# A chunked linear recurrence with its chunk loops written out and its transposes in another order

## The reference, cut to what matters

```
r, k, v, w, a, b: (batch 4, heads 8, seq 768, dim 40)
for t in range(768):
    y[t]  = r_t @ state                       # state: 40 x 40 per batch and head
    Sa    = state @ a_t
    state = state * w_t - outer(Sa, b_t) + outer(v_t, k_t)
x   = y as (3072, 320)
P   = exp(x @ w_gate - max), normalised by rows and columns 8 times
x   = sum over 8 experts of P[:, e] * (relu(x @ w1[e]) @ w2[e])    # inner width 1024
out = elu(x @ w_in) @ w_out                                        # inner width 2048
```

## Time and profile before

| | |
|---|---|
| Median of 3 runs | 2286.55 us (2280.87 to 2287.19) |
| The profiled execution | 2284.05 us, of which the span is 2282.2 |
| Recurrence | from 0 to about 504 us |
| Gate and experts, second layer | about 512 to 2282 us |
| TensorE busy | 2223.5 us (97% of the span) |
| VectorE, ScalarE, GpSimd busy | 1121.3, 617.4, 176.5 us |

### The profile page before, as it was taken

One profiled execution on the slowest core, in us unless ns is written; L12 is line 12 of the kernel. 1 busy time (PEld: TensorE's weight loads), 2 busy tenths in 40 slices (PEclk: granted clock), 3 DMA queues, 4 the chain that ended last, 5 costly groups with the idle time before them and its releaser, 6 DMA issues.

```text
span 2282.2 us, 37511 instructions
## 1 busy us (share of the span) xinstructions
PE 2223.5 (97%) x14896; PEld 2003.6 (88%) x14896; DVE 1121.3 (49%) x2067; ACT 617.4 (27%) x1113; POOL 176.5 (8%) x194
## 2 busy tenths in 40 slices
PE   7999999979999999999999999999999999999999
PEld 6898888868899998998998998998998998999998
DVE  6776676764363433333333333333333334766665
ACT  3433333323221121221221221221221222433333
POOL 3433333320000000000000000000000000000000
PEclk9999999999999999999999999999999999999999
DMA  5332332322000000100000000000100000000001
GB/s 98 60 59 48 62 60 52 57 55 82 26 26 1 26 26 1 26 26 1 26 26 1 26 15 12 26 2 25 26 1 26 26 1 26 26 1 26 1 12 58
DMA packets 184149, 67.54 MB, mean 30 GB/s; under 512 B 153008, under 2 KB 174000, under 8 KB 183984
## 3 DMA queue, kind: packets, MB, share of 16 engines
q1 hardware_dynamic: 183984, 65.04, 12.2%
HBM read 57.16 MB, written 7.86 MB: 28 GB/s over the span
## 4 chain that ended last, share of the span: by engine, by line
PE 90%; issue 5%; POOL 3%; DVE 2%; ACT 0%; POOLq 0%; DVEq 0%; ACTq 0%
PE up L1099 39%; PE yps L1114 12%; PE yps L1113 12%; PE yps L1112 12%; PE misc L920 4%; PE yps L878 2%; PE up L893 1%; POOL kt L549 1%; PE up L854 1%; PE up L878 1%; PE up L901 1%; PE misc L913 1%; POOL bt L547 1%; PE yps L834 1%; DVE winv L1189 1%
## 5 line engine op out<-in xcount | busy, mean ns | idle before, releaser
L1457 DVE SCALAR_TENSOR_TENSOR hl<-up,hh 128x512 fp32r<-128x512 f32 x384 | 265.5, 691 | 875.7 <-ACT hh L675 875.6
L1114 PE MATMUL yps<-w2h,hl 128*128 128x320 f32 x1920 | 592.7, 309 | 0.0
L1113 PE MATMUL yps<-w2l,hh 128*128 128x320 f32 x1920 | 591.7, 308 | 0.0
L1112 PE MATMUL yps<-w2h,hh 128*128 128x320 f32 x1920 | 591.2, 308 | 0.0
L675 ACT ACTIVATE hh<-up 128x512 fp32r<-128x512 f32 x384 | 229.5, 598 | 1104.2 <-PE up L1099 1104.2
L1099 PE MATMUL up<-xh,w1h 128*128 128x512 f32 x960 | 381.9, 398 | 11.5 <-issue 6.4
L1099 PE MATMUL up<-xl,w1h 128*128 128x512 f32 x960 | 379.5, 395 | 0.0
L1112 PEld LDWEIGHTS yps<-w2h,hh 128*128 128x128 f32 x1920 | 360.6, 188 | 20.4
L1113 PEld LDWEIGHTS yps<-w2l,hh 128*128 128x128 f32 x1920 | 360.5, 188 | 20.4
L1099 PE MATMUL up<-xh,w1l 128*128 128x512 f32 x960 | 377.0, 393 | 0.0
L1114 PEld LDWEIGHTS yps<-w2h,hl 128*128 128x128 f32 x1920 | 360.3, 188 | 0.0
(11 more groups left out here) (189 smaller groups left out, 2211.4 us busy)
## 6 DMA issues: line engine op xcount, KB each, us to landing
w_raw<-in_moe_w SPq DMA_DIRECT2D x16, 640.0 KB, 5.7
w_raw<-in_moe_w SPq DMA_DIRECT2D x16, 512.0 KB, 3.9
w_raw<-in_moe_w SPq DMA_DIRECT2D x32, 128.0 KB, 4.2
wp<-in_w SPq DMA_DIRECT2D x24, 160.0 KB, 2.6
rp<-in_r SPq DMA_DIRECT2D x24, 160.0 KB, 2.5
vp<-in_v SPq DMA_DIRECT2D x48, 80.0 KB, 2.4
raw<-in_a SPq DMA_DIRECT2D x24, 160.0 KB, 3.2
raw<-in_b SPq DMA_DIRECT2D x24, 160.0 KB, 3.5
```

The lines of the kernel that those rows point to most:

```text
L1112: nc.tensor.matmul(o, hh[:, k % RING, c], w2h[buf][:, f, :], start=(f == 0), stop=False)
L1113: nc.tensor.matmul(o, hh[:, k % RING, c], w2l[buf][:, f, :], start=False, stop=False)
L1114: nc.tensor.matmul(o, hl[:, k % RING, c], w2h[buf][:, f, :], start=False, stop=(f == NF - 1)).then_inc(s_down, 1)
L1457: nc.vector.scalar_tensor_tensor(out=hl[:, k % RING, :], in0=up[:, k % UP_BANKS, :], scalar=0.0, in1=hh[:, k % RING, :].bitcast(F32), op0= ...
```

## The change

The loops over chunks 1 to 4 become Python loops on all five engines, so that every chunk is straight code and waits compare with constants. The transposes of a no longer use a job bank but `pw`. That leaves nine jobs with banks in an octet, so the banks' turns differ from octet to octet, which a class now counts. v's four transposes are split, two ahead of the second round and two ahead of the fourth; r's go from ahead of the fourth round to behind it, in front of a's; a_state goes from behind k's transposes to in front of them. ScalarE's copies keep their order.

```
+class Jobs(Count):
+    def __init__(self):
+        super().__init__(0)
+        self.slot, self.user = 0, [0, 0]
+    def take(self):
+        slot, before = self.slot, self.user[self.slot]
+        self.slot, self.user[slot] = 1 - slot, self.next()
+        return slot, before
...
-            with nc.sync.Fori(0, NG - 1) as g:
+            for g in range(0, NG - 1):
                 load_chunk(g)
...
-            with nc.gpsimd.Fori(1, NG - 1) as g:      # likewise scalar, tensor, vector
+            for g in range(1, NG - 1):
                 chunk(g)
...
-            def job(tj, dst, src):
-                n = tj.n
-                act.wait_ge(c_tj, tj.next())
-                nc.scalar.activation(dst, src(pt[:, n % 2, :]), ACT.Copy).then_inc(c_ta, 1)
+            def job(tj, dst, src, bank=None):
+                if bank is None:
+                    bank = pt[:, tj.take()[0], :]
+                else:
+                    tj.next()
+                act.wait_ge(c_tj, tj.now())
+                nc.scalar.activation(dst, src(bank), ACT.Copy).then_inc(c_ta, 1)
...
-                    channels(tj, a_t)
+                    channels(tj, a_t, pw)
...
             def job_bank(tj):
-                n = tj.n
-                wait(pe, c_ta, tj.next() - 2)
-                return pt[:, n % 2, :]
+                slot, before = tj.take()
+                wait(pe, c_ta, before)
+                return pt[:, slot, :]
...
+            def slots_of_pairs(bank, tile, some):
+                for p in some:
+                    ins = nc.tensor.transpose(bank[:, p * P:(p + 1) * P], slots(tile, p), ident[:])
+                return ins
...
             def a_by_channels(tj, g, bb):
                 pe.wait_ge(c_at, g * B + bb + 1)
-                by_channels(tj, at)
+                for p in range(PAIRS):
+                    ins = nc.tensor.transpose(pw[0:PR, p * P:(p + 1) * P], pair_of(at, p), ident[:])
+                tj.next()
+                ins.then_inc(c_tj, 1)
...
             def value_query(tj, buf):
-                slot = tj.n % 2
-                tj.next()
-                pe.wait_ge(c_ta, tj.next() - 2)
+                slot, before = tj.take()
+                wait(pe, c_ta, max(before, tj.take()[1]))
...
                 round_of(n_b, x_b)
                 if following:
                     w_by_tokens(tj, *following)
-                    v_by_channels(tj, *following)
+                    pe.wait_ge(c_rv[1 - buf], fills(*following) * 3 * 16)
+                    v_bank = job_bank(tj)
+                    slots_of_pairs(v_bank, vp[:, 1 - buf], range(PAIRS // 2))
...
                 if following:
-                    by_channels(tj, rp[:, 1 - buf])
+                    slots_of_pairs(v_bank, vp[:, 1 - buf], range(PAIRS // 2, PAIRS)).then_inc(c_tj, 1)
                 pe.wait_ge(c_za, o * ROUNDS + 3)
                 round_of(n_b, z_b)
                 if following:
+                    by_channels(tj, rp[:, 1 - buf])
                     a_by_channels(tj, *following)
...
                     b_by_channels(tj, *following)
                     b_done = tj.now()
-                    k_by_channels(tj, *following)
-                    k_done = tj.now()
                     if not empty or bb + 1 == B:
                         pe.wait_ge(c_zd, o + 1)
                         pe.wait_ge(c_ta, a_done)
                         a_state(*following)
+                    k_by_channels(tj, *following)
+                    k_done = tj.now()
```

More of the change, by code:

```diff
@@ L734, in right_side, with channels @@
                                      ACT.Copy, scale=-1.0).then_inc(c_xc, 1)
-            def channels(tj, dst):
-                job(tj, dst[0:PR], pairs(PR))
+            def channels(tj, dst, bank=None):
+                job(tj, dst[0:PR], pairs(PR), bank)
             def value_query(tj):
@@ L769, in chunk @@
             def chunk(g, last=False):
-                tj = Count(g * (B * JOBS))
-                tj.n = T0
                 for bb in range(B):
-                    octet(tj, g, bb, (g, bb + 1) if bb + 1 < B else None if last else (g + 1, 0), last)
+                    octet(first, g, bb, (g, bb + 1) if bb + 1 < B else None if last else (g + 1, 0), last)
             act.wait_ge(s_sel, 1)
@@ L780, in _ @@
                                          .broadcast_to([P, PAIRS, 2, width]), ACT.Copy, scale=0.0).then_inc(c_zero, 1)
-            first = Count(0)
+            first = Jobs()
             channels(first, r_t[:, 0])
@@ L784, in _ @@
             previous(first, 0, 0)
-            for tile in (a_t, b_t, k_t):
-                channels(first, tile)
+            channels(first, a_t, pw)
+            channels(first, b_t)
+            channels(first, k_t)
             rough(0, 0)
@@ L790, in _ @@
             chunk(0)
-            with nc.scalar.Fori(1, NG - 1) as g:
+            for g in range(1, NG - 1):
                 chunk(g)
@@ L849, in by_channels @@
                 ins.then_inc(c_tj, 1)
+            def slots_of_pairs(bank, tile, some):
+                for p in some:
+                    ins = nc.tensor.transpose(bank[:, p * P:(p + 1) * P], slots(tile, p), ident[:])
+                return ins
             def slots_by_channels(tj, tile):
[L852 to L859, removed]
+                slots_of_pairs(job_bank(tj), tile, range(PAIRS)).then_inc(c_tj, 1)
             def a_by_channels(tj, g, bb):
                 pe.wait_ge(c_at, g * B + bb + 1)
-                by_channels(tj, at)
+                for p in range(PAIRS):
+                    ins = nc.tensor.transpose(pw[0:PR, p * P:(p + 1) * P], pair_of(at, p), ident[:])
+                tj.next()
+                ins.then_inc(c_tj, 1)
             def b_by_channels(tj, g, bb):
@@ L1000, in octet @@
                 y_by_head(bt[:, buf], rs_t, last=True).then_inc(c_yj, 1)
+            tj = Jobs()
             def chunk(g, last=False):
-                tj = Count(g * (B * JOBS))
-                tj.n = T0
                 for bb in range(B):
                     octet(tj, g, bb, (g, bb + 1) if bb + 1 < B else None if last else (g + 1, 0), last)
-            tj = Count(0)
             pe.wait_ge(c_const, 1)
@@ L1013, in _ @@
             by_channels(tj, rp[:, 0])
-            v_by_channels(tj, 0, 0)
+            slots_by_channels(tj, vp[:, 0])
             w_by_tokens(tj, 0, 0)
@@ L1026, in _ @@
             chunk(0)
-            with nc.tensor.Fori(1, NG - 1) as g:
+            for g in range(1, NG - 1):
                 chunk(g)
@@ L1353, in _ @@
             assert dd.n == LINKS
-            with nc.vector.Fori(1, NG - 1) as g:
+            for g in range(1, NG - 1):
                 dd = Count(g * LINKS + START)
```

## The result

The changed kernel's median is 2262.44 us (2261.70 to 2263.82, 5 runs), against 2285.29 for the one before with two further runs. The ratio is 0.9911, with a 95% interval of 0.9900 to 0.9921. The profiled execution took 2262.37 us with a span of 2260.6, where 2260.1 was forecast: 21.6 us less than before, against 22.1. For the median 2264.4 was forecast. One execution of a later kernel, the one with one more copy on ScalarE, took 7459 us at a mean granted clock of 0.35, and its ratio leaves that one out.

What follows compares the result with a forecast made beforehand. TensorE's queue was taken to bound the whole program. Gains of 13.8 + 7.5 + 0.2 + 0.6 = 22.1 us gave a span of 2260.1 and a median of 2264 us, range 2257 to 2273.

Steps and rivals of the forecast that it cites:

- The edges: Chunk loop's three jumps back on TensorE: writing the loops out removes 13.8 us of stalls and slow clock.
- The rival that the branch is not the cause: Loop edges: the stall belongs to something that stays; gain only 8.6 us, time 2278; chance 0.02.
- Straight code on all five engines: Rival, chunks 1 to 4: fresh instruction fetches starve the engines; no change, or slower at 2293; chance 0.07.
- The octet: Fourth octet of chunk 0 and 16 of chunks 1 to 4: 0.44 us sooner each, 7.5 us in all.
- The 0.06 ahead of Z: Fourth round: with two of v's transposes before it instead of r's four, it comes 0.06 us sooner.
- Z: Zero point of the octet's timings: start of the fourth and last of an octet's correction rounds on TensorE (L920).
- the 0.08 lost behind it: r and a behind the fourth round: zf by bt, r_t and sa_t products and b each 0.08 us later.
- 0.48 per queued copy over 0.60: ScalarE's r_t, a_t, sa_t copies: each follows by 0.48 us; waiting the whole 0.60 would make b 0.20 later.
- r_t at Z+0.45 with the same delay of 0.69: r's transposes start at Z+0.45; ScalarE's r_t copy forecast at Z+1.10, by sa_t's 0.69 us delay after zf's first transpose.
- The rival was near: ScalarE becomes what TensorE waits for, at r_t and sa_t products: 0.20 us per octet, gain 18, time 2268; chance 0.10.
- The forecast's own sign of being wrong: Wrong if TensorE's products of r_t and sa_t wait for ScalarE's sa_t by more than 0.1 us.
- The small terms: Octets 1 to 3 of chunk 0: 0.2 us in all; three octets of the last chunk: 0.2 each, 0.6 us.

## Why the prediction was right

**The edges.** Forecast 13.8 us. The three long distances of the earlier trace rows are gone, and the kernel with TensorE's loop alone written out shows the term by itself, 13.85 us over the 16 looped octets. Its median is 13.1 us below that of the kernel before on its chip, and with all five loops written out 11.5. (The spans of the profiled executions, 14.3 and 15.3 us lower, also hold what the start and the expert layers vary by.) The rival that the branch is not the cause fell with it. Straight code on all five engines cost next to nothing: its octets are even at 19.84, but for the one told of at the end.

**The octet.** Forecast 0.44 each, 7.5 us for 17. From the profiles: before, a plain octet took 19.85 us; after, 17 of them took 330.15 us from 78.98, 19.42 each, the odd one of 19.76 included. That is 7.3 us. The step that makes it is a_state ahead of k, and it was named. It alone gives 0.43 in one kernel, and undoing it takes 0.40 away in another. The 0.06 ahead of Z and the 0.08 lost behind it nearly cancel, and both were measured as the forecast's own working had them.

**ScalarE.** The forecast took 0.48 per queued copy over 0.60 and was right by 0.01. One reading was off by 0.04 without harm: r_t at Z+0.45 with the same delay of 0.69 is Z+1.14 and not Z+1.10, though 1.10 is what was measured. The rival was near: one more copy in that queue costs 0.45 us an octet. In the last chunk it came true in part. The forecast's own sign of being wrong, that the products of r_t and sa_t wait for sa_t by more than 0.1 us, is seen there, with 0.79; before the change it was 0.69 already, which the forecast had not looked at.

**The small terms.** Octets 2 and 3 of chunk 0 were to gain 0.06 each ahead of Z. They lost 0.02 (19.02 us for 19.00). The overlooked step is mt's transposes. They wait for b_t's copy, which now comes 0.08 later behind Z. Timeline of TensorE and then ScalarE at the end of the third octet, kernel after and then kernel before:

```profile
77.84 0.66 PE L868 MATMUL up<-ident,kt 128*128 128x128 f32 x4 [0.17 <-POOL kt L562]
78.44 0.54 PE L1008 MATMUL up<-ident,mt 104*104 104x104 f32 x4
```

```profile
77.70 0.60 ACT L727 ACTIVATE b_t<-up 104x512 f32<-104x512 f32 x1 [1.87 <-PE up L868]
```

```profile
77.75 0.54 PE L989 MATMUL up<-ident,mt 104*104 104x104 f32 x4
```

```profile
77.01 0.60 ACT L711 ACTIVATE b_t<-up 104x512 f32<-104x512 f32 x1 [1.97 <-PE up L854]
```

b_t is done at 78.30 and mt starts at 78.44; before, b_t was done at 77.61 and mt started at 77.75, each time 0.14 behind the copy. From k to mt it is 0.60 us instead of the 0.52 before (k was at 77.23), and 0.08 less 0.06 are the 0.02 lost. That this is the bank's wait was read from the profile and not tried by itself. The last chunk gave 3 x 0.17 = 0.5 us for the 0.6 forecast. That near agreement is luck: the exchange gave 0.35 an octet, and the moves of v and r lost 0.18 of it.

**What was not forecast.** The first octet took 22.13 us, where it had taken 21.49. Its 16 products at 25.24 took 2.88 us in the chain of waits, against 2.27 in the kernel before and 1.98 later in the recurrence. The trace's record of the granted clock begins only at 27.39 us of the span here, and at 26.10 in the kernel before, so that the clock of these products isn't shown. That a slow stretch at the start ended later fits the numbers, but it is an inference. In all profiles the first octet took between 19.25 and 23.03 us, and in two executions of the same kernel, whose clock records begin at 26.02 and 20.38 us, it took 21.34 and 19.25. So the difference lies within what executions vary by. What follows the last n products took 0.7 us less (1794.4 us for 1795.2), and between the profiles that varies from 1792.9 to 1795.9.

The forecast put the median 2.5 us above the profiled execution. It was 0.07 above it, so the median came out 2.0 us below the forecast, well inside its range. The clock was to be 1.00 from 30 to 500 us; it is until 481.4, shortly before the recurrence ends, and then at the lower level for 13.7 us, as it was before at the recurrence's end (from 504.0).

Sum from the profiles: 13.8 + 7.3 - 0.64 - 0.04 + 0.5 + 0.7 = 21.6 us.

## What to carry to other kernels

Where one engine is the bound, take the distances between one recurring group of it: a distance that stands out gives the price of a jump, with the slow clock behind it, more surely than the jump's own record. Write out the loop of that engine alone; the others' loops were free here, where TensorE was the bound. In an order written by hand, look for a group that stands behind a wait it doesn't share, and put it in front: one exchange of two neighbours gave 0.43 us of the octet's 0.45, while a new bank, split transposes and their bookkeeping gave nothing in the middle chunks and lost 0.18 us an octet in the last. Then fill the pauses by their measured length, in transposes of 0.11 us, and not by whole jobs.

## What the runs showed of the hardware

**Only TensorE's jump was dear.** Its record was 3.3 to 3.9 us for each jump taken and 0.08 for each not taken. The other four engines' jumps were recorded with 0.04 to 0.07 us each, and their loops, written out, moved nothing. TensorE's loop body is also the longest (over its four octets some 1,900 products and weight loads, by the earlier trace rows), and whether the price comes from the engine or from the length of the body was not tried.

**The order of two waits.** Of two waits ahead of one instruction on VectorE, it mattered which stood first in the program: with the event that comes last put first, every octet was 0.07 us shorter (19.33 against 19.40). This was tried at one place.

**A delay in straight code.** In the six profiles with every loop written out and the waits in their old order, the thirteenth octet (from 253.57 us in the changed kernel) was 0.35 to 0.36 us longer. Timeline of VectorE there, kernel after:

```profile
261.86 0.49 DVE L1278 TENSOR_TENSOR z_b<-xf,misc 128x320 bf16<-128x320 f32 x1 [1.43 <-PE misc L936]
```

It stood idle 1.43 us; in the other octets the same instruction has 1.07:

```profile
222.70 0.49 DVE L1278 TENSOR_TENSOR z_b<-xf,misc 128x320 bf16<-128x320 f32 x1 [1.07 <-PE misc L936]
```

With VectorE still looped it was absent, and with the waits swapped as well. It might be a joint between two pieces of fetched code, just behind the wait. The Trainium skill (Runtime: NRT & Kernel Launch, "Instruction fetch mechanics") has code arrive in 16 KiB blocks and calls the crossing mostly hidden. Whether such a crossing is the cause here was not tried and stays open; it is 0.36 us in all.
